# State products that alternate between the array's halves, and another order of the first tile's loads

## The reference, cut to what matters

```python
kv  = einsum('bhsd,bhse->bhde', k, v)          # 8 batches, 8 heads, 576 rows, head size 64: the state
out = einsum('bhsd,bhde->bhse', q, kv)
x   = out / sqrt(mean(out*out) + 1e-6) * g_norm # per head; then (4608, 512)
h   = x @ w_in                                  # 512 -> 2048
y   = (max(h,0) + alpha*min(h,0)) @ w_out       # 2048 -> 512
# then 8 experts, one per token by argmax(y @ w_gate): relu(y @ w1[e]) @ w2[e],
# scaled by the softmax weight and by sigmoid(y @ w_output_gate)[e]
```

## Time and profile before

| | us |
|---|---|
| median of 3 runs | 1520.47 (1520.08 to 1521.70) |
| the profiled execution | 1524.66 |
| its span | 1522.80 |
| TensorE busy | 1493.7 (98%) |
| VectorE busy | 716.5 (47%) |
| ScalarE busy | 490.9 (32%) |

### The profile page before, as it was taken

One profiled execution on the slowest core, in us unless ns is written; L12 is line 12 of the kernel. 1 busy time (PEld: TensorE's weight loads), 2 busy tenths in 40 slices (PEclk: granted clock), 3 DMA queues, 4 the chain that ended last, 5 costly groups with the idle time before them and its releaser, 6 DMA issues.

```text
span 1522.8 us, 27026 instructions
## 1 busy us (share of the span) xinstructions
PE 1493.7 (98%) x8463; PEld 1313.5 (86%) x8464; DVE 716.5 (47%) x1779; ACT 490.9 (32%) x994; POOL 126.9 (8%) x143
## 2 busy tenths in 40 slices
PE   7899999999999999999999999999999999999997
PEld 6789898999999999999999999887888888888886
DVE  2585545565545455545555554654122114444411
ACT  2343232323232323223232322234233224444422
POOL 1000000000000000000000000121111111111111
PEclk9899999999999999999999999999999999999999
DMA  9342121102112101202110000444114114444410
GB/s 193 103 118 73 33 73 33 42 1 73 33 53 52 36 8 36 70 22 53 33 42 2 22 1 22 98 133 147 43 56 132 42 42 149 154 144 148 150 48 31
DMA packets 100515, 104.49 MB, mean 69 GB/s; under 512 B 55296, under 2 KB 75920, under 8 KB 100434
## 3 DMA queue, kind: packets, MB, share of 16 engines
q1 hardware_dynamic: 91618, 80.99, 19.1%
q0 software_dynamic: 7872, 21.09, 4.4%
q10 hardware_dynamic: 944, 1.33, 0.4%
HBM read 84.04 MB, written 20.65 MB: 69 GB/s over the span
## 4 chain that ended last, share of the span: by engine, by line
PE 92%; DVE 3%; DMA 2%; ACT 2%; issue 1%; POOL 0%; SPq 0%; ACTq 0%; POOLq 0%
PE psAcc L1296 25%; PE psH L1284 25%; PE psAcc L1412 14%; PE psH L1391 14%; PE psO L1401 2%; PE psO L1238 2%; PE psO L1210 2%; PE psY L1262 2%; PE psQ L1372 1%; PE psQ L1224 1%; PE psY L1248 1%; PE psY L1256 1%; DMA AR<-in_v_dram 1%; DMA AR<-rows,uid 1%; DVE W L921 1%
## 5 line engine op out<-in xcount | busy, mean ns | idle before, releaser
L1296 PE MATMUL psAcc<-W,XG 128*128 128x512 f32 x1728 | 439.5, 400 | 0.0
L1284 PE MATMUL psH<-XG,W 128*128 128x384 f32 x2304 | 436.3, 337 | 0.5 <-DVE W L923 0.5
L1284 PEld LDWEIGHTS psH<-XG,W 128*128 128x128 f32 x2304 | 408.7, 188 | 15.7 <-issue 0.7
L1296 PEld LDWEIGHTS psAcc<-W,XG 128*128 128x128 f32 x1728 | 315.6, 189 | 59.8 <-DVE XG L957 0.2
L668 ACT ACTIVATE XG<-AR 128x128 fp32r<-128x128 f32 (+1 forms) x384 | 132.2, 364 | 648.9 <-DVE AR L953 646.7
L950 DVE TENSOR_SCALAR AR<-psH,acol 128x384 f32<-128x384 f32 x192 | 118.5, 617 | 320.4 <-PE psH L1284 319.7
L1391 PE MATMUL psH<-W,XG 128*128 (+1 forms) x996 | 250.5, 400 | 1.3 <-DVE W L931 1.1
L1412 PE MATMUL psAcc<-W,XG 128*128 (+1 forms) x984 | 244.3, 397 | 0.0
L1412 PEld LDWEIGHTS psAcc<-W,XG 128*128 128x128 f32 x984 | 183.3, 190 | 37.6 <-issue 0.3
L1391 PEld LDWEIGHTS psH<-W,XG 128*128 128x128 f32 x996 | 180.9, 188 | 38.7 <-DVE W L931 1.5
L1114 DVE TENSOR_TENSOR XG<-psO,XG 128x512 fp32r<-128x512 f32 x82 | 56.6, 690 | 219.8 <-ACT XG L726 219.8
(11 more groups left out here) (192 smaller groups left out, 923.0 us busy)
## 6 DMA issues: line engine op xcount, KB each, us to landing
AR<-in_moe_w_dram SPq DMA_DIRECT2D x68, 512.0 KB, 4.7
AR<-in_k_dram SPq DMA_DIRECT2D x16, 576.0 KB, 5.4
rows<-AR SPq DMA_DIRECT2D x36, 256.0 KB, 2.3
AR<-in_q_dram SPq DMA_DIRECT2D x32, 256.0 KB, 3.1
AR<-in_v_dram SPq DMA_DIRECT2D x14, 576.0 KB, 6.8
AR<-in_moe_w_in_dram SPq DMA_DIRECT2D x16, 256.0 KB, 2.8
AR<-in_moe_w_out_dram SPq DMA_DIRECT2D x16, 256.0 KB, 3.1
AR<-in_v_dram ACTq DMA_DIRECT2D x2, 576.0 KB, 9.6
```

The costliest lines, as they stand in the source:

```text
L1284: mm = pe.matmul(psH[f % 2][:, 0:TILE], w_in_v[:, wp, cc, f * P:(f + 1) * P], xT[:, b, xp, cc, :], start=(cc == 0 and (wp, xp) == PARTS[0] ...
L1296: mm = pe.matmul(psAcc[m][:, :], gT[:, f % 2, gp, m * P:(m + 1) * P], w_out_v[:, wp, f, :], start=(f == 0 and (gp, wp) == PARTS[0]), stop= ...
```

## The change

In `k_times_v` the loop over the halves r becomes the innermost, so matmuls alternate between them. `pad` moves into the memory of `tab` and `first_qT` into the space of v of state 1, so that the second half of `stage1` is free from the start. SyncE issues block 1 right behind block 0, state 2 ahead of the gates, then block 2, q of the second tile, block 3, state 3. `dense_high(1)` on ScalarE comes ahead of `x_evacuate`. gcol and arow get a semaphore of their own (`first_in`), and the wait for the gates goes to the first `logits`. 24 transposes of the identity stand ahead of the first `x_transpose`.

```diff
--- before.py
+++ after.py
@@ -137,13 +137,12 @@
         meta = sb("meta", [P, TG, META])
         umeta = sb("umeta", [P, 2, 2])
         uid = sb("uid", [P, 2], I32)
-        pad = stage1[:, 1, 0:SLOTS // P].bitcast(I32)
         padmeta = sb("padmeta", [1, META])
 
 
         k_first = AR[:, A2:A2 + KN].rearrange("p (h j d) -> p h j d", h=HH, j=KVJ)
         v_first = AR[:, A2 + KN:A2 + 2 * KN].rearrange("p (h j d) -> p h j d", h=HH, j=KVJ)
-        first_qT = [qT] + [stage1[:, 1, m * DM:(m + 1) * DM].rearrange("p (c n) -> p c n", c=CH)
+        first_qT = [qT] + [AR[:, A2 + (3 + m) * DM:A2 + (4 + m) * DM].rearrange("p (c n) -> p c n", c=CH)
                            for m in range(TG - 1)]
         tail_yT = [yT, qT, AR[:, A2 + 2 * KN - DM:A2 + 2 * KN].rearrange("p (c n) -> p c n", c=CH)]
 
@@ -161,7 +160,9 @@
         OFFSET, FIRST, REST, GROUP, AGAIN, TURN, PARITY, NEXT, AFTER, COUNT = range(FIELDS)
         tcol = sb("tcol", [P, FIELDS + 3])
         COLS = UNITS + 1
-        tab = sb("tab", [1, FIELDS, COLS], I32)
+        tab_mem = sb("tab_mem", [P, FIELDS * COLS], I32)
+        tab = tab_mem[0:1, :].rearrange("p (f u) -> p f u", f=FIELDS)
+        pad = tab_mem[:, 0:SLOTS // P]
 
         psAcc = [pb(f"psAcc{m}") for m in range(3)]
         psH = [pb("psH0"), pb("psH1")]
@@ -175,7 +176,7 @@
         consts = sem("consts")
         small_in = sem("small_in")
         alpha_T = sem("alpha_T")
-        alpha_in = sem("alpha_in")
+        first_in = sem("first_in")
         stage_in = [sem("stage_in0"), sem("stage_in1")]
         dense_hi = sem("dense_hi")
         dense_hi_0 = sem("dense_hi_0")
@@ -348,22 +349,22 @@
             load_rows(sp, k, 0, 1, k_first, kv_in_1)
             load_q(0, 0, first=True)
             load_dense(0)
+            load_dense(1)
             for r in range(2):
-                sp.dma_start(gcol[r * D:(r + 1) * D, :], g_norm.rearrange("(d o) -> d o", o=1)).then_inc(small_in, 16)
-            sp.dma_start(arow[:, :], alpha.rearrange("(f p) -> f p", p=P)).then_inc(alpha_in, 16)
+                sp.dma_start(gcol[r * D:(r + 1) * D, :], g_norm.rearrange("(d o) -> d o", o=1)).then_inc(first_in, 16)
+            sp.dma_start(arow[:, :], alpha.rearrange("(f p) -> f p", p=P)).then_inc(first_in, 16)
+            load_kv(2, 1, 0)
             for r, src in enumerate((w_gate, w_og)):
                 sp.dma_start(wg[:, :, r * E:(r + 1) * E],
                              src.rearrange("(c p) e -> p c e", p=P)).then_inc(small_in, 16)
-            load_kv(2, 1, 0)
+            load_dense(2)
             sp.dma_start(rows[N:N + 1, 0:DM].rearrange("o (p n) -> p (o n)", n=META),
                          meta[0:DM // META, 0, :]).then_inc(small_in, 16)
             sp.dma_start(rows[N:N + 1, DM:DM + META], padmeta[:, :]).then_inc(small_in, 16)
             load_q(0, 1)
-            sp.wait_ge(o_mm, TG)
-            load_dense(1)
+            load_dense(3)
             load_kv(3, 1, 1)
-            load_dense(2)
-            for f in range(3, FC):
+            for f in range(4, FC):
                 load_dense(f)
 
             def tile(i, c, before=True, ahead=True, kv=False):
@@ -525,7 +526,7 @@
 
             pool.wait_ge(y_saved, 16 * TG * (TILES - 1))
             pool.wait_ge(meta_saved, 16 * (TILES - 1))
-            pool.wait_ge(small_in, 96)
+            pool.wait_ge(small_in, 64)
 
             def gather(r, n):
                 pool.wait_ge(ids_in[r], 16 * n + 16)
@@ -653,11 +654,11 @@
             root(0)
             act.wait_ge(alpha_T, 1)
             nc.scalar.activation(acol[:, :], psY[:, 0:FC], ACT.Copy).then_inc(alpha_T, 1)
-            act.wait_ge(small_in, 96)
+            act.wait_ge(first_in, 48)
+            dense_high(1)
             for j in range(TG):
                 x_evacuate(0, 0, j)
             kv_evacuate(2, 1, 0)
-            dense_high(1)
 
             def step(i, c, f):
                 t = 3 * i + c
@@ -937,7 +938,7 @@
             normalise(0)
             for j in range(TG):
                 scale_rows(0, j)
-            dve.wait_ge(small_in, 96)
+            dve.wait_ge(first_in, 48)
             dve.wait_ge(alpha_T, 2)
             for j in range(TG):
                 x_low(0, 0, j)
@@ -1205,8 +1206,8 @@
                 bank = FIRST_KV[n] if isinstance(n, int) and n < 3 else psO
                 kr, vr = (k_first, v_first) if isinstance(n, int) and n == 1 else (k_rows, v_rows)
                 for c in range(2):
-                    for r in range(2):
-                        for j in range(KVJ):
+                    for j in range(KVJ):
+                        for r in range(2):
                             mm = pe.matmul(bank[r * D:(r + 1) * D, c * D:(c + 1) * D], kr[0:KVP, 2 * c + r, j, :],
                                            vr[0:KVP, 2 * c + r, j, :], start=(j == 0), stop=(j == KVJ - 1),
                                            tile_position=(0, r * D))
@@ -1257,6 +1258,8 @@
                 mm.then_inc(y_tr, 1)
 
             def logits(t, m):
+                if t == 0 and m == 0:
+                    pe.wait_ge(small_in, 64)
                 pe.wait_ge(yT_set, 3 * t + m + 1)
                 for cc in range(CH):
                     mm = pe.matmul(psY[:, 0:2 * E], yT[:, cc, :], wg[:, cc, :], start=(cc == 0), stop=(cc == CH - 1))
@@ -1316,9 +1319,11 @@
             q_transpose(0, 0, 2)
             q_times_kv(0, 0, 1, 2)
             q_times_kv(0, 0, 2, 2)
-            pe.wait_ge(alpha_in, 16)
+            pe.wait_ge(first_in, 48)
             pe.transpose(psY[:, 0:FC], arow[:, :], ident[0:FC, 0:FC]).then_inc(alpha_T, 1)
             pe.wait_ge(alpha_T, 2)
+            for _ in range(24):
+                pe.transpose(psQ[:, 0:P], ident[:, :], ident[:, :])
             for j in range(TG):
                 x_transpose(0, j)
             k_times_v(2)
```

## The result

The changed kernel takes 1509.37 us (median of 5 runs, 1506.57 to 1511.66), the kernel before 1521.70 in the same comparison (1520.08 to 1523.93). The ratio is 0.9918, with a 95% interval of 0.9902 to 0.9935: faster by 0.8%, or some 12 us. The forecast was 1507.4 us, with a range of 1502.5 to 1512.5.

A forecast was written before the change was run, and what follows sets the result against it. TensorE was taken as the bound, with 92% of the chain. 10.0 us from steady state products and 3.1 from the first tile sum to 13.1, taking the median from 1520.47 to 1507.4 us, range 1502.5 to 1512.5.

The forecast's parts named there:

- Part 1: Twelve steady `k_times_v` calls: alternating halves cuts first to last start from 2.25 to 1.42 us, 10.0 us in all.
- The step that carried it: In `k_times_v`, the halves are two streams of 59 ns a pass, and at a turn both run.
- upper bound of 10.6 us: Most the twelve steady `k_times_v` calls could gain, if both halves start at once and nothing is lost.
- B: In `k_times_v` halves overlap, but each visit pays the exposed 0.10 us again; total 1513.2 us; chance 0.04.
- C: Overlap does not repeat with close turns; a steady `k_times_v` call stays at 2.40 us, total 1517.4; chance 0.04.
- D: Each turn in `k_times_v` stops the old half and pays the exposed load: 3.8 us a call, total 1539; chance 0.04.
- Part 2: First tile: new load order and shorter state products start the q product earlier, 3.1 us, between 1.3 and 4.4.
- The term that was mis-sized: First tile: state 3's load lands at 40.7 us, from 4.72 MB at 240 GB/s plus 1.5 us for small loads.
- the late case: First tile: VectorE's split of block 1 comes late, dense 3 is issued at 34 us, state 3 lands at 42.5.
- rival A: The start gains nothing: state 3 lands at 43 to 44 us behind waiting loads; total 1510.5 us; chance 0.13.
- The step behind the landing: First tile: with block 2 there early and ScalarE free, the q product starts 3.5 us after state 3 lands.
- the prediction's own signs: State product 3 at 39.5 to 42.5 us, block 2's split before 35, first output group not after 48.

The follow-up runs named there:

- the three profiles: The changed kernel, profiled once and then twice more with nothing altered: 1509.37, 1511.00 and, in one run, 1514.12 us.
- the second profile: The changed kernel profiled again with nothing altered, to see what varies by itself: 1511.00 us, ratio 0.9920 to the kernel before.
- the third: The changed kernel profiled once more with nothing altered: 1514.12 us in one run.
- the other two profiles: The kernel before, profiled twice more with nothing altered: medians 1522.98 and 1521.99 us.
- the second comparison: The changed kernel timed again, unaltered, together with the kernel before: 1511.00 against 1521.99 us, ratio 0.9920.
- the one with the longer product: The changed kernel with the old loop order in `k_times_v`: 1523.82 us, ratio 1.0007 to the kernel before.

## Why the prediction was right, and where it was not

**Part 1, 10.0 us: right, at 10.3.** A call was to fall from 2.25 to 1.42 between first and last start; it fell to 1.40, 0.856 less, twelve times. The step that carried it, that the turn in the earlier trace rows shows two independent streams, holds at every pass now. (Its upper bound of 10.6 us does not follow from its own terms: 12 x (2.25 - 1.40) is 10.2, which the measured 10.3 just passes.) The issue of passes every 29 ns was no limit. VectorE did not become the bound. Rivals B, C and D fell: a call takes neither 1.9 nor 2.4 nor 3.8 us. The rule of the Trainium skill ("TensorE: Matmul & The Clock Gate", Part 3: a weight load overlaps matmuls in flight only across row groups) does not hold here for column halves: with the same 96 rows, a pass every 29 ns instead of every 58.

**Part 2, 3.1 us: its size was wrong, measured 0.6,** outside its own bounds of 1.3 to 4.4. Step by step: state product 1 shorter by 1.45 (forecast 1.46); alpha's transpose at 20.90, 22.11 and 22.89 in the three profiles (forecast near 22; it waited for the load in the last two); `dense_high(1)` free; the 24 transposes 4.50 us in the first profile (forecast 2.8 to 5.5) and neither a gain nor a loss; first hidden group at 31.09 (29.5 to 33.8); from state 3's landing to the q product 3.58 us (3.5). The term that was mis-sized is the landing, forecast at 40.7 and measured at 43.34, 41.33 and 43.91, mean 42.9. It was worked out from bytes, as if the transfer engines were never idle from block 0 on. They idle from about 31 to 33 us (24 GB/s), because state 3 stands behind block 3, which waits for VectorE's split of block 1, which comes behind VectorE's work on x. In the second profile, with the early landing of 41.33, these two us have 101 GB/s; in the third, with 43.91, they have 20, and the next two 42. By an estimate, 2 us at 24 instead of 240 GB/s are 1.8 of the 2.6 us by which 43.34 misses 40.7; the rest is a mean rate under the assumed 240. I had that chain as the late case (42.5) and as rival A, and took the engines' rate as the likely one. Moving state 3 ahead of it gave 38.77.

The step behind the landing was right. From the landing to the second tile it is 74.3 us on the mean of three profiles, 77.1 before: 2.8 us gained, by the copy that no longer waits for block 2. The landing itself takes 2.1 of these back (mean 42.9 against 40.7 before): state 3 is issued 0.5 us later on the mean, and takes 9.5 instead of 7.8 us from there, with block 3 ahead of it. By the prediction's own signs the start failed: the first output group was not to come after 48 us and came at 48.62, 46.60 and 49.18, state product 3 started after 42.5 in two of three, and ScalarE's split of block 2 started at 35.72, 34.69 and 37.00, where it was to start before 35.

A second error sat in the comparison: 47.34 for the q product before was one draw; the other two profiles have 46.86 and 46.17. So rival A (the start gains nothing, for the reason that it gave) came closer to what happened in the start than the forecast; the measured median lies between 1507.4, the forecast, and A's 1510.5. The direction and the range held because the steady part is large. That the first comparison's 12.3 us are so near to the forecast's 13.1 is in part luck: the stages account for 10.3 + 0.6 = 10.9, as the second comparison's 11.0 does, and the rest lies in the scatter.

Of the clock: by the Trainium skill ("TensorE: Matmul & The Clock Gate", Part 4) transposes should not count as activity. The windows of the changed kernel show the clock at 0.50 from 23.15 to 26.55 with nothing but these fp32 transposes on TensorE, behind 1.94 us of idle, and at 1.00 from there on. Here the clock rose on them alone.

## What to carry to other kernels

If matmuls use one half of the array's columns, let consecutive ones alternate between the halves. Here each half was a stream of its own, and with long runs in one half only about three passes a turn overlapped (0.18 us, at 0.058 us a pass). Look for the evidence in the trace of before, at a place where the program already turns from one half to the other. When a load is moved, count the waits that stand in front of it in its queue and not only the bytes: a load whose buffer is free should not stand behind one that waits for computed data.

## What was not expected of the hardware

A shorter burst at the low clock need not save time. State product 3 took 2.83 us instead of 4.07, but the clock rose at 50.4 instead of 47.0 us; from the landing of state 3 to the second tile the changed kernel took 74.04 to 74.64 us, the one with the longer product 73.66. This is one profile against three, and the cause of the earlier rise was not tested.

The gain of a turn between the halves can be counted. A call took 2.61, 2.25, 1.56 and 1.40 us from first to last start with 1, 3, 7 and 23 turns: 0.18 us less for each turn as long as the runs in one half are of six passes or more.
